# Gated linear attention with two MLP layers on one core: near score groups of the two lanes in neighbouring slots, one PSUM bank per lane

## The chip, the cores and the metric

The kernel runs on one core of a Trainium2 chip. The metric is the device time of one execution in microseconds; three executions of the kernel before gave 985.92 us (median; 984.63 to 988.6).

## The reference

```python
B, H, S, D = 4, 8, 768, 48
# attention: a state of D x D per batch and head, decayed row by row and added to
for t in range(S):
    state = alpha[:, :, t, :, None] * state + k[:, :, t] (outer) v[:, :, t]
    y[:, :, t] = q[:, :, t] @ state
# then, with the heads side by side: 3072 tokens, model 384, hidden 2048
x = y.transpose(0, 2, 1, 3).reshape(3072, 384)
h = x @ w_in;  x = (h - tanh(h)) @ w_out                                  # first MLP
h = x @ w_in;  out = (max(h, 0) + alpha * min(h, 0)) @ w_out              # second MLP
```

## The kernel before

The sequence is cut into 6 tiles of 128 steps (C); a tile with the 4 batches has 512 tokens. Tile by tile two kinds of work are interleaved: the MLP of one tile and the attention of the next. The 6 tiles of the first MLP come first (five with the attention of the next tile beside them), then the 6 of the second MLP with nothing beside them.

**The MLP.** An MLP tile is a list of 32 half slots (LAYER; here "slots"), each with 9 matmuls of 128x512 on TensorE (float32 in three products of a high and a low half). An "in" slot (0, 1, then every even one up to 28) makes one block of 128 hidden rows in the bank `ph`; an "out" slot (every odd one from 3, and 30) adds one to `acc`. After an "in" slot ACT makes the tanh, DVE the difference g (`make_g`), ACT the high half, DVE the low half (`g_low`).

**The attention.** Within a tile of 128 steps the decay is handled in 7 levels of halving (l = 1 to 7). Level by level POOL multiplies the left halves of k (`grow`, in place in `k_t`) and makes the tree of products of alpha (`product`), and DVE multiplies the right halves of q (`q_first` for the elements by alpha itself, `grow` for the levels) by totals that ACT has copied to the bank `py` (`copy_left_totals`). TensorE makes 8 groups of scores (e = 1 to 8). Groups 1 to 6 are "near": blocks of 32x32, written into one of two banks `ps`, in turns by e. DVE moves each under a mask into `near` (`mask`), and POOL places them in `prob`. Groups 7 and 8 are copied by ACT. Then come the outputs (Y, of `prob` and v and of the state), the transposes of k (KT) and the new state (ST). Group e needs k at level e - 2, q at level e - 1 and, before, mask e - 2, since that mask reads the bank that e writes.

There are 16 pairs of heads (X). A **lane** is half of them: 8 pairs (XL), 2 batches. The first tile, which has nothing to hide behind, is done lane by lane, each with two banks of scores of its own. The other five do both lanes in one group: 64 matmuls of the program for a near group, 128 in the records, since each float32 matmul is recorded twice, and as many weight loads.

**The order** beside the MLP is a table written by hand. `E_SLOT` gives the slot of each score group, and `beside()` puts masks, growth and copies of totals at or behind it. Each engine walks the same table: layer work of slot h, then the table's work of slot h. On DVE an "in" slot does `make_g` first, and an "out" slot does its `g_low` behind the table's work. What matters here:

```python
E_SLOT = {1: 4, 2: 6, 3: 9, 4: 12, 5: 15, 6: 18, 7: 21, 8: 24}
    for side in range(2):
        slots[E_SLOT[2] + 1 + side].insert(0, ("q_first", side))
```

So group 2 stands at slot 6, the two halves of `q_first` at slots 7 and 8, and group 3, which needs both, at slot 9. In the first MLP tile DVE, ACT and SP also split 12 blocks of weights (`weights`, an extra piece in each odd slot). The loads are issued by SP: `load_tile(a)` (lines 329 to 346) waits, then loads q, alpha, k and v of a tile in this order.

## Time and profile before

| what | us |
|---|---|
| three executions, median (lowest, highest) | 985.92 (984.63, 988.6) |
| the profiled execution, its own time | 993.91 |
| its span (first to last instruction) | 992.1 |
| first MLP tile with attention beside it (47.9 to 154.5) | 106.60 |
| the three in the loop | 97.40, 97.30, 95.60 |
| the fifth, without a new state | 86.70 |
| an MLP tile alone | 65.70 |

The tiles are stretches of the trace between the first matmuls of slot 0. A page of the profile gives busy time by engine (PE is TensorE's matmuls, PEld its weight loads), the granted clock in tenths, and groups of instructions by source line with their mean duration and the idle time ahead of them. "issue" is idle time for which no wait shows. A group of score matmuls in the trace has the line 432 (near), 427 (group 7) or 420 (group 8).

### The profile page before, as it was taken

How to read it: one execution, taken by the hardware profiler on the slowest of the kernel's cores; microseconds unless marked ns; L12 is line 12 of the kernel's file. 1: busy time of each engine (PE TensorE's matmuls, PEld its weight loads, DVE VectorE, ACT ScalarE, POOL GpSimd, SP SyncE). 2: the span in 40 equal slices, each digit the busy share in tenths (PEclk: the TensorE clock that was granted, in tenths of full speed). 3: DMA queues.
4: the chain of work that ended last, by engine and by line, in shares of the span. 5: the costliest groups of instructions: out<-in, count | busy, mean ns of one | idle time of the engine just before them, and what ended most of it. 6: DMA issues, size and time to landing. Idle time of an engine off the chain costs nothing.

```text
span 992.1 us, 23757 instructions
## 1 busy us (share of the span) xinstructions
PE 938.4 (95%) x10296; PEld 769.4 (78%) x10296; DVE 556.4 (56%) x695; ACT 319.2 (32%) x527; POOL 191.3 (19%) x186
## 2 busy tenths in 40 slices
PE   4688999899989998999999999999999999999998
PEld 3567778678768876887888888888888888888887
DVE  8857755564456445645653445555555555555553
ACT  4633453235323432443254452121121221211211
POOL 6422322241124112501430442000000000000000
PEclk7699999899989998999999999999999999999999
DMA  5462133004200410051004401010010010100000
GB/s 156 111 216 65 34 72 122 2 2 112 83 2 2 124 71 3 2 155 39 3 2 154 166 1 64 0 62 2 0 63 0 0 63 0 63 0 0 32 1 32
DMA packets 28999, 51.67 MB, mean 52 GB/s; under 512 B 2032, under 2 KB 19440, under 8 KB 26864
## 3 DMA queue, kind: packets, MB, share of 16 engines
q1 hardware_dynamic: 28912, 50.35, 16.7%
q8 instruction: 75, 1.23, 0.5%
q14 instruction: 12, 0.10, 0.0%
HBM read 40.90 MB, written 9.44 MB: 51 GB/s over the span
## 4 chain that ended last, share of the span: by engine, by line
PE 93%; issue 4%; DVE 2%; ACT 1%; DMA 1%; DVEq 0%; SPq 0%
PE ph L577 41%; PE acc L586 14%; PE acc L587 13%; PE acc L588 13%; PE ps L432 4%; PE py L489 1%; PE ps L420 1%; PE ps L489 1%; PE py L485 1%; PE ps L530 1%; DVE q_w L793 1%; PE ps L485 1%; DMA q_early<-q 1%; PE acc L432 1%; PE ps L427 1%
## 5 line engine op out<-in xcount | busy, mean ns | idle before, releaser
L757 ACT ACTIVATE g_hi<-g 128x512 fp32r<-128x512 f32 x192 | 121.1, 631 | 447.7 <-PE acc L588 382.9
L939 DVE TENSOR_TENSOR g_lo<-g,g_hi 128x512 fp32r<-128x512 f32 x192 | 142.1, 740 | 188.0 <-ACT g_hi L757 187.3
L586 PE MATMUL acc<-g_lo,w_hi 128*128 128x512 f32 x576 | 230.8, 401 | 0.0
L587 PE MATMUL acc<-g_hi,w_lo 128*128 128x512 f32 x576 | 225.7, 392 | 0.0
L588 PE MATMUL acc<-g_hi,w_hi 128*128 128x512 f32 x576 | 225.6, 392 | 0.0
L577 PE MATMUL ph<-x_hi,w_lo 128*128 128x512 f32 x576 | 166.9, 398 | 5.0 <-issue 2.8
L577 PE MATMUL ph<-x_hi,w_hi 128*128 128x512 f32 x576 | 164.7, 394 | 0.2 <-issue 0.2
L577 PE MATMUL ph<-x_lo,w_hi 128*128 128x512 f32 x576 | 164.5, 394 | 0.0
L925 DVE TENSOR_TENSOR g<-ph,g 128x512 f32<-128x512 f32 x96 | 66.2, 689 | 135.8 <-ACT g L738 135.5
L577 PEld LDWEIGHTS ph<-x_hi,w_lo 128*128 128x128 f32 x576 | 107.4, 190 | 29.2 <-issue 7.1
L586 PEld LDWEIGHTS acc<-g_lo,w_hi 128*128 128x128 f32 x576 | 108.9, 189 | 25.6 <-issue 2.2
L577 PEld LDWEIGHTS ph<-x_lo,w_hi 128*128 128x128 f32 x576 | 109.8, 191 | 23.7 <-issue 0.4
L577 PEld LDWEIGHTS ph<-x_hi,w_hi 128*128 128x128 f32 x576 | 109.7, 190 | 23.4
L588 PEld LDWEIGHTS acc<-g_hi,w_hi 128*128 128x128 f32 x576 | 109.1, 189 | 23.6
L587 PEld LDWEIGHTS acc<-g_hi,w_lo 128*128 128x128 f32 x576 | 109.1, 189 | 21.4
L1006 POOL TENSOR_TENSOR k_t<-k_t,tree 128x512 f32<-128x512 f32 x72 | 83.1, 1172 | 187.4 <-PE ps L432 145.9
L931 DVE TENSOR_SCALAR g<-ph,slope 128x512 f32<-128x512 f32 x96 | 72.0, 750 | 58.3 <-PE ph L577 58.3
L738 ACT ACTIVATE g<-ph 128x512 f32<-128x512 f32 x96 | 57.4, 598 | 137.7 <-PE ph L577 137.4
L432 PEld LDWEIGHTS ps<-q_w,k_t 128*32 128x32 f32 x4096 | 40.7, 112 | 37.8 <-issue 36.8
L432 PE MATMUL ps<-q_w,k_t 128*32 128x32 f32 x4096 | 45.2, 201 | 26.1 <-issue 20.6
L934 DVE SCALAR_TENSOR_TENSOR g<-ph,g 128x512 f32<-128x512 f32 x96 | 66.4, 692 | 3.3
L804 DVE TENSOR_TENSOR q_w<-q_w,py 64x1024 f32<-64x1024 f32 (+1 forms) x56 | 64.8, 1157 | 2.0 <-PE ps L432 1.1
(109 smaller groups left out, 599.6 us busy)
## 6 DMA issues: line engine op xcount, KB each, us to landing
v_t<-v SPq DMA_DIRECT2D x6, 1024.0 KB, 5.3
a_t<-alpha SPq DMA_DIRECT2D x5, 1024.0 KB, 4.9
k_t<-k SPq DMA_DIRECT2D x5, 1024.0 KB, 4.9
x<-x_out SPq DMA_DIRECT2D x6, 768.0 KB, 4.2
x_in<-x SPq DMA_DIRECT2D x6, 768.0 KB, 5.1
q_w<-q SPq DMA_DIRECT2D x10, 384.0 KB, 7.2
out<-prob SPq DMA_DIRECT2D x5, 768.0 KB, 3.8
w_raw<-w_in SPq DMA_DIRECT2D x16, 192.0 KB, 3.5
```

The lines of the kernel that those rows point to most:

```text
L432: mm = pe.matmul(at[t, NEAR * i0:NEAR * i0 + NEAR], k_t[:, x * C + t.start:x * C + t.stop], moving(x, t), start=True, stop=True)
L577: mm = pe.matmul(ph[:, f % 2, :], w[:, f, kt * 128:(kt + 1) * 128], x[:, kt, :], start=(j == 0 and kt == 0), stop=(j == 2 and kt == KT - 1))
L586: pe.matmul(acc[:, m, :], w_hi[:, f, part], g_lo[:, f % 2, :], start=(f == 0), stop=False)
L587: pe.matmul(acc[:, m, :], w_lo[:, f, part], g_hi[:, f % 2, :], start=False, stop=False)
L588: mm = pe.matmul(acc[:, m, :], w_hi[:, f, part], g_hi[:, f % 2, :], start=False, stop=(f == NF - 1))
L757: act.activation(g_hi[:, f % 2, :], g[:, f % 2, :], ACT.Copy).then_inc(g_hi_made, 1)
L804: dve.tensor_tensor(to, right, left_for_q(lane, l, rows), ALU.mult).then_inc(q_last if to_end else q_grown[set_of(lane)], 1)
L925: dve.tensor_tensor(g[:, f % 2, :], ph[:, f % 2, :], g[:, f % 2, :], ALU.subtract).then_inc(g_made, 1)
L931: dve.tensor_scalar(g[:, f % 2, :], ph[:, f % 2, :], 0.0, slope[:, f:f + 1], ALU.min, ALU.mult).then_inc(g_part, 1)
L934: dve.scalar_tensor_tensor(out=g[:, f % 2, :], in0=ph[:, f % 2, :], scalar=0.0, in1=g[:, f % 2, :], op0=ALU.max, op1=ALU.add).then_inc(g_m ...
L939: dve.tensor_tensor(g_lo[:, f % 2, :], g[:, f % 2, :], g_hi[:, f % 2, :].bitcast(F32), ALU.subtract).then_inc(g_lo_made, 1)
L1006: pool.tensor_tensor(left, left, right_totals.to_broadcast([128, XL * nb, half]), ALU.mult).then_inc(done, 1)
```

## The change

The five later tiles also work lane by lane where the scores are near. Each lane has one bank (`ps[:, lane, :]`) for all its score groups, in place of one bank for odd and one for even e. Groups 1 to 6 become two groups of half the size in neighbouring slots (lane 0 at slot h, lane 1 at h + 1); groups 7 and 8 stay in one slot, as two halves. Group 1 moves from slot 4 to 3, group 2 from 6 to 5. Masks, `q_first` and `grow` of a lane stand one slot behind its group, each of half the size; both halves of `q_first` are now in one slot. Since a lane has one bank, group e waits for mask e - 1 of its lane, and group 8 for the copies of group 7 of its lane. Copies of totals, products and placements stay together. Counters become per-lane counters. The load of q waits for the last Y of the tile before (`y_done`) rather than for `q_copied` and `q_last`.

```diff
-E_SLOT = {1: 4, 2: 6, 3: 9, 4: 12, 5: 15, 6: 18, 7: 21, 8: 24}
+E_SLOT = {1: 3, 2: 5, 3: 9, 4: 12, 5: 15, 6: 18, 7: 21, 8: 24}
...
     for e, h in E_SLOT.items():
-        slots[h].append(("scores", e))
+        for lane in range(LANES):
+            at = h + (lane if e <= 6 else 0)
+            slots[at].append(("scores", lane, e))
+            if e == 2:
+                slots[at + 1].append(("q_first", lane, 0))
+            if e > 2:
+                slots[at + 1].append(("grow", lane, e - 1))
+            if e <= 6:
+                slots[at + 1].append(("mask", lane, e))
         if e > 2:
-            slots[h].append(("left", e - 1))
-            slots[h + 1].append(("grow", e - 1))
-        if e <= 6:
-            slots[h + (1 if e == 1 else 2)].append(("mask", e))
-    for side in range(2):
-        slots[E_SLOT[2] + 1 + side].insert(0, ("q_first", side))
...
+            slots[h].append(("left", 0, e - 1))
...
-        def scores_of(lane, e):
-            if lane is None:
-                return ps[:, (e - 1) % 2, :]
-            return lane_scores[lane][(e - 1) % 2][:, 0:512 if e == 8 else 256]
+        def scores_of(a, lane, e):
+            bank = lane_scores[lane][(e - 1) % 2] if is_tile(a, 0) else ps[:, lane, :]
+            return bank[:, 0:512 if e == 8 else 256]
...
             def load_tile(a):
 
-                n = a - 1
-                if is_tile(a, 1):
-                    for lane in range(LANES):
-                        sp.wait_ge(scored[lane], SCORED)
-                else:
-                    sp.wait_ge(q_copied, 2 * n)
-                    sp.wait_ge(q_last, 2 * n)
+                sp.wait_ge(y_done, B * a)
                 for hh in range(2):
...
-                sp.wait_ge(y_done, B * a)
                 sp.dma_start(a_t[:, :], alpha[bass.ds(a * 128, 128), :]).then_inc(ld_a[LANES], 16)
...
                 if e == 2:
-                    pe.wait_ge(state_made, STATES * a)
-                    pe.wait_ge(k_grown[LANES], K_GROWN * n + K_PARTS)
-                    group(None, 2, plain(q_w, 1))
+                    pe.wait_ge(k_grown[lane], K_GROWN * a + 1)
+                    pe.wait_ge(masked[lane], MASKED * a + 1)
+                    group(a, lane, 2, plain(q_w, 1))
                     return
-                pe.wait_ge(k_grown[LANES], K_GROWN * n + K_PARTS * (e - 2))
-                pe.wait_ge(q_grown[LANES], Q_GROWN * n + 2 * (e - 1))
-                pe.wait_ge(masked[LANES], MASKED * n + e - 2)
-                if e == 8:
-                    pe.wait_ge(copied[LANES], FAR_COPIES * n + 4)
-                group(None, e, grown(e - 1))
+                pe.wait_ge(k_grown[lane], K_GROWN * a + e - 2)
+                pe.wait_ge(q_grown[lane], Q_GROWN * a + 2 * (e - 1))
+                if e < 8:
+                    pe.wait_ge(masked[lane], MASKED * a + e - 1)
+                else:
+                    pe.wait_ge(copied[lane], COPIED * a + 4)
+                group(a, lane, e, grown(e - 1))
```

How the instructions stand before and now, at three places. The rows are those of the attention beside the first MLP tile; the loop has the same order. `x32` after a row counts equal instructions of the program, and names in brackets are the counters waited for (`masked_lane0` and so on belong to a lane, names without a lane to both).

TensorE, group 3 at slots 9 and 10, before:

```order
L432 MATMUL ps<-q_w,k_t 32x32 [waits masked,q_grown,k_grown]
L432 MATMUL ps<-q_w,k_t 32x32 x63
L577 MATMUL ph<-x_hi,w_lo 128x512 [waits g_made,w_lo_made]
L577 MATMUL ph<-x_hi,w_lo 128x512 x2
L577 MATMUL ph<-x_hi,w_hi 128x512 x3
L577 MATMUL ph<-x_lo,w_hi 128x512 x3
```

and now:

```order
L426 MATMUL ps<-q_w,k_t 32x32 [waits masked_lane0,q_grown_lane0,k_grown_lane0]
L426 MATMUL ps<-q_w,k_t 32x32 x31
L573 MATMUL ph<-x_hi,w_lo 128x512 [waits g_made,w_lo_made]
L573 MATMUL ph<-x_hi,w_lo 128x512 x2
L573 MATMUL ph<-x_hi,w_hi 128x512 x3
L573 MATMUL ph<-x_lo,w_hi 128x512 x3
L426 MATMUL ps<-q_w,k_t 32x32 [waits masked_lane1,q_grown_lane1,k_grown_lane1]
L426 MATMUL ps<-q_w,k_t 32x32 x31
```

The 64 matmuls in a row became 32, nine matmuls of the MLP, and 32.

DVE, slots 6 to 8 (from group 2 to the end of `q_first`), before:

```order
L925 TENSOR_TENSOR g<-ph,g 128x512 [waits g_part]
L793 TENSOR_TENSOR q_w<-q_w,a_t 64x16x64 [waits scored,ld_a]
L793 TENSOR_TENSOR q_w<-q_w,a_t 64x16x64
L939 TENSOR_TENSOR g_lo<-g,g_hi 128x512 [waits g_hi_made]
L914 TENSOR_TENSOR w_lo<-w_raw,w_hi 128x768 [waits w_lo_made,w_hi_made]
L925 TENSOR_TENSOR g<-ph,g 128x512 [waits g_part]
L793 TENSOR_TENSOR q_w<-q_w,tree 64x16x64 [waits scored,tree_made]
L793 TENSOR_TENSOR q_w<-q_w,tree 64x16x64
L814 TENSOR_TENSOR near<-ps,near_masks 128x512 [waits masked,scored]
```

and now, slots 3 to 6 (the row of `w_lo` is in the first MLP tile alone):

```order
L922 TENSOR_TENSOR g_lo<-g,g_hi 128x512 [waits g_hi_made]
L897 TENSOR_TENSOR w_lo<-w_raw,w_hi 128x768 [waits w_lo_made,w_hi_made]
L908 TENSOR_TENSOR g<-ph,g 128x512 [waits g_part]
L798 TENSOR_TENSOR near<-ps,near_masks 128x256 [waits scored_lane0,placed_lane0,masked_lane0]
L798 TENSOR_TENSOR near<-ps,near_masks 128x256 [waits scored_lane1,placed_lane1,masked_lane1]
L922 TENSOR_TENSOR g_lo<-g,g_hi 128x512 [waits g_hi_made]
L897 TENSOR_TENSOR w_lo<-w_raw,w_hi 128x768 [waits w_lo_made,w_hi_made]
L908 TENSOR_TENSOR g<-ph,g 128x512 [waits g_part]
L779 TENSOR_TENSOR q_w<-q_w,a_t 64x8x64 [waits scored_lane0,ld_a]
L779 TENSOR_TENSOR q_w<-q_w,a_t 64x8x64
L779 TENSOR_TENSOR q_w<-q_w,tree 64x8x64 [waits tree_made]
L779 TENSOR_TENSOR q_w<-q_w,tree 64x8x64
```

The second half of `q_first` no longer stands behind the `make_g` of slot 8; the first mask of lane 0 stands behind the `w_lo` of slot 3 and the `make_g` of slot 4.

DVE, slots 18 to 20 (behind group 6), now:

```order
L908 TENSOR_TENSOR g<-ph,g 128x512 [waits g_part]
L790 TENSOR_TENSOR q_w<-q_w,py 64x8x4x16 [waits q_grown_lane0,left_copied,scored_lane0]
L790 TENSOR_TENSOR q_w<-q_w,py 64x8x4x16
L805 COPY_PREDICATED near<-near_masks,ps 128x16x16 [waits masked_lane0,scored_lane0]
L922 TENSOR_TENSOR g_lo<-g,g_hi 128x512 [waits g_hi_made]
L897 TENSOR_TENSOR w_lo<-w_raw,w_hi 128x768 [waits w_lo_made,w_hi_made]
L908 TENSOR_TENSOR g<-ph,g 128x512 [waits g_part]
L790 TENSOR_TENSOR q_w<-q_w,py 64x8x4x16 [waits q_grown_lane1,left_copied,scored_lane1]
L790 TENSOR_TENSOR q_w<-q_w,py 64x8x4x16
L805 COPY_PREDICATED near<-near_masks,ps 128x16x16 [waits masked_lane1,scored_lane1]
```

The growth for group 7 of lane 1 now stands behind the `make_g` of slot 20; both lanes' growth stood ahead of it.

## Rows read from the trace of the kernel before

**Rows 1.** Page, part 1: busy time, share, instructions.
```profile
PE 938.4 (95%) x10296; PEld 769.4 (78%) x10296; DVE 556.4 (56%) x695; ACT 319.2 (32%) x527; POOL 191.3 (19%) x186
```
**Rows 2.** Windows by MLP tile: us, busy by engine (xinstructions), PEclk, DMA share, GB/s.
```profile
251.90:349.20 97.30, 91.73 (x1456) 74.29 (x1456) 52.24 (x61) 34.06 (x60) 25.42 (x25) 0.96 0.17 48
...
531.50:597.20 65.70, 65.70 (x290) 53.98 (x289) 29.31 (x33) 32.74 (x50) 25.70 (x14) 1.00 0.36 121
```
**Rows 3.** Timeline of PE, second loop tile, slots 9, 10: start, us, work, [idle before].
```profile
277.61 1.26 PE L432 MATMUL ps<-q_w,k_t 128*32 128x32 f32 x124 [1.83 <-DVE q_w L793]
281.31 0.32 PE L432 MATMUL ps<-q_w,k_t 128*32 128x32 f32 x4 [2.44 <-issue]
281.56 1.65 PE L577 MATMUL ph<-x_hi,w_lo 128*128 128x512 f32 x3
...
288.58 0.84 PE L577 MATMUL ph<-x_hi,w_lo 128*128 128x512 f32 x3
```
**Rows 4.** Timeline of DVE at the same place.
```profile
275.02 2.46 DVE L793 TENSOR_TENSOR q_w<-q_w,tree 64x1024 f32<-64x1024 f32 x2
```
**Rows 5.** DMA queues in 278 to 281.3 us: packets, MB, share.
```profile
q8 instruction: 1, 0.02, 2.5%
```
**Rows 6.** Page, part 3: DMA queues of the whole span.
```profile
q8 instruction: 75, 1.23, 0.5%
```
**Rows 7.** Windows at the place of rows 3, columns as in rows 2.
```profile
284.00:287.50 3.50, 3.50 (x10) 2.73 (x9) 1.06 (x2) 0.60 (x1) 0.92 (x2) 0.50 0.00 0
```
**Rows 8.** Timeline of PE: the same group in the third loop tile and in the fifth tile.
```profile
378.33 0.32 PE L432 MATMUL ps<-q_w,k_t 128*32 128x32 f32 x4 [2.16 <-issue]
378.58 1.65 PE L577 MATMUL ph<-x_hi,w_lo 128*128 128x512 f32 x3
...
384.93 0.84 PE L577 MATMUL ph<-x_hi,w_lo 128*128 128x512 f32 x3
...
470.14 1.29 PE L432 MATMUL ps<-q_w,k_t 128*32 128x32 f32 x128 [1.80 <-issue]
```
**Rows 9.** Timeline of PE: idle times of the first MLP tile.
```profile
66.94 0.38 PE L432 MATMUL ps<-q_w,k_t 128*32 128x32 f32 x19 [2.24 <-issue]
...
75.18 0.54 PE L432 MATMUL ps<-q_w,k_t 128*32 128x32 f32 x38 [2.64 <-issue]
75.64 0.53 PE L586 MATMUL acc<-g_lo,w_hi 128*128 128x512 f32 x1
...
79.38 0.88 PE L577 MATMUL ph<-x_hi,w_lo 128*128 128x512 f32 x3
...
85.48 1.29 PE L432 MATMUL ps<-q_w,k_t 128*32 128x32 f32 x128 [1.79 <-issue]
...
111.88 0.39 PE L432 MATMUL ps<-q_w,k_t 128*32 128x32 f32 x23 [2.22 <-issue]
...
127.36 1.97 PE L420 MATMUL ps<-q_w,k_t 128*64 128x128 f32 x32 [1.35 <-issue]
```
**Rows 10.** Timeline of PE: an "in" slot and a group, then an "out" slot.
```profile
260.45 0.84 PE L577 MATMUL ph<-x_hi,w_lo 128*128 128x512 f32 x3
...
263.81 0.50 PE L586 MATMUL acc<-g_lo,w_hi 128*128 128x512 f32 x1
```
**Rows 11.** Lines by form, DVE, 0 to 48 us: half-size operations.
```profile
L804 DVE TENSOR_TENSOR q_w<-q_w,py 64x512 f32<-64x512 f32 x6 | 4.1, 683 | 0.1
L821 DVE COPY_PREDICATED near<-near_masks,ps 128x256 f32<-128x256 uint32 x4 | 2.1, 513 | 0.2
```
**Rows 12.** Timeline of DVE, then PE: behind slots 20 and 21, second loop tile.
```profile
312.78 0.71 DVE L821 COPY_PREDICATED near<-near_masks,ps 128x512 f32<-128x512 uint32 x1
...
313.47 1.10 PE L427 MATMUL ps<-q_w,k_t 128*32 128x64 f32 x64
```
**Rows 13.** Timeline of ACT, first MLP tile: arrival of weights.
```profile
66.84 0.85 ACT L765 ACTIVATE w_hi<-w_raw 128x768 fp32r<-128x768 f32 x1 [4.58 <-DMA w_raw<-w_out]
```
**Rows 14.** Timeline of SP's DMA issues, second loop tile.
```profile
329.06 1.40 SPq L339 DMA_DIRECT2D q_w<-q  x2
```

More of the change, by code:

```diff
@@ L447, in first_scores @@
                     pe.wait_ge(ld_q[lane], 32)
-                    group(lane, 1, plain(q_early, 0))
+                    group(0, lane, 1, plain(q_early, 0))
                     return
@@ L451, in first_scores @@
                 if l == 2:
-                    group(lane, 2, plain(q_early, 1))
+                    group(0, lane, 2, plain(q_early, 1))
                     pe.wait_ge(pads_cleared, 2)
@@ L554, in attention @@
             def attention(work, a):
-                for what, i in work:
+                for what, lane, i in work:
                     if what == "scores":
-                        scores(a, i)
+                        scores(a, lane, i)
                     if what == "Y":
@@ L685, in attention @@
                 n = a - 1
-                for what, i in work:
+                for what, lane, i in work:
                     if what == "left":
@@ L824, in mask @@
                         [128, count, nb, half]),
-                    scores_of(lane, e).rearrange("p (h n t) -> p h n t", h=count, t=half)).then_inc(done, 1)
+                    scores_of(a, lane, e).rearrange("p (h n t) -> p h n t", h=count, t=half)).then_inc(masked[lane], 1)
             def place_near_first(lane):
@@ L846, in first_tile @@
                         dve.wait_ge(scored[lane], 1)
-                        mask(lane, 1)
+                        mask(0, lane, 1)
                         continue
@@ L858, in first_tile @@
                     if l < LEVELS - 1:
-                        mask(lane, l + 1)
+                        mask(0, lane, l + 1)
                     elif lane > 0:
@@ L1027, in attention @@
                 n = a - 1
-                for what, e in work:
+                for what, lane, e in work:
                     if what != "scores" or e == 2:
```

237 lines of the change are left out of this document (113 added, 124 removed).

## The prediction

> **What bounds the kernel now.** I read the page first. TensorE is busy for 95% of the span; DVE, the next engine, for 56% [rows 1]. Windows by MLP tile then show that TensorE is not at its limit everywhere: a tile with nothing beside it takes 65.70 us and is all busy, a loop tile takes 97.30 us with 91.73 busy, so 5.6 us are idle, and its mean clock is 0.96 [rows 2]. The change adds and removes no arithmetic on TensorE, so what it can give is in the idle time and in the lost clock. The timeline of TensorE shows where they lie in a loop tile: all at group 3. TensorE waits 1.83 us for DVE's `q_first`, runs 124 of the group's 128 matmuls, stands still for another 2.44 us for which no wait shows ("issue"), and then runs two slots slowly [rows 3].
>
> The first wait has a plain cause: the second half of `q_first` takes 2.46 us on DVE and could start only at 275.02, behind the `make_g` of slot 8 [rows 4].
>
> The second stop is the arrival of code, as I read it. One packet of the instruction queue falls into it [rows 5]. Over the span the queue moved 75 packets and 1.23 MB, 16.4 KB each [rows 6], against 20,592 recorded matmuls and weight loads [rows 1], about 275 for a packet. A near group is 256 such records in 1.26 us, nearly a whole packet's worth. From the end of the wait to the last four matmuls 3.70 us pass (281.31 less 277.61) [rows 3]; if a packet needs up to that long from its cause to its use, TensorE reads such a group faster than the next packet can come. The Trainium skill ("Runtime: NRT & Kernel Launch", Instruction fetch mechanics) speaks of blocks of 16 KiB, or 256 instructions, and says that crossing into one is "mostly hidden". The size agrees with the rows above; the second half speaks against my reading, and what follows from it is a rival below.
>
> The third loss is the clock. Behind these stops it is 0.50, the 1.2 GHz level [rows 7]. The two slots behind group 3 take 7.02 us (281.56 to 288.58) [rows 3] in place of 4.1 (two of 65.70 / 32) [rows 2], so 2.9 us are lost.
>
> **What goes.** I count by tile in the profiled execution.
> - `q_first`. 1.83 us in each of the three loop tiles [rows 3], 1.79 in the first MLP tile [rows 9], 1.80 in the fifth [rows 8]: 9.1 us. Now lane 0's four pieces start behind the `make_g` of slot 6. DVE is free of a `make_g` 1.4 us behind the slot (slot 20: 312.78, and the slot ended a slot's 2.1 us before 313.47 [rows 12]); four pieces of half size cost about 0.68 each [rows 11] (the nearest form), 2.7 us, so they end 4.1 us behind slot 6. TensorE needs them after half a group (0.65) and three slots (6.2), at 6.8. Lane 1 ends at 4.1 + 0.45 (mask) + 2.7 = 7.3, needed at 6.8 + 0.65 + 2.05 = 9.5. Both are covered by more than 2 us of MLP work. Without that cover the wait would be what it was.
> - Code. 2.44 in the first and second loop tile (the first has the rows of the second) [rows 3], 2.16 in the third [rows 8], and in the first MLP tile 2.24, 2.64 and 2.22, each inside a near group [rows 9]: 14.1 us. Groups are now 128 records with a slot between: 256 records span at least two half groups and a slot, 1.3 + 2.05 = 3.3 us. Against 3.7 that leaves 0 to 0.4 us at an unlucky place. I take 0.5 us for the whole kernel.
> - Clock. 2.9 us in the second loop tile, 2.2 (6.35 less 4.1) in the third [rows 8], about as much in the first, 1.7 in the first MLP tile (75.64 to 79.38, less 2.05) [rows 9]: 9.1 us.
> - Group 8 in the first MLP tile waited 1.35 us for a late growth [rows 9]. Each lane's growth is now half as long, and lane 1 has lane 0's matmuls as cover: 1.3 us go.
>
> **What comes.**
> - Group 7, lane 1. It waits for the growth and for mask 6 of its lane, both behind the `make_g` of slot 20. In the trace DVE is free of that `make_g` at 312.78 [rows 12]. Two growths of 0.68 and a mask of 0.45 to 0.51 [rows 11] end at 314.6. Group 7 began at 313.47, and its second half could begin at 314.0 (half of 1.10 on) [rows 12]. So TensorE waits 0.6 us, in five tiles: 3.1 us. What stands behind it on DVE, `g_low`, is not needed for two slots.
> - More seams. A near group costs 3.36 us with its slot [rows 10], 1.31 more than the slot; the 128 matmuls themselves need no more than 1.26. The seam is 0.05 at least; from the form of the half groups nothing shows it. I take 0.1 and bound it by 0.25. Six more per tile, five tiles: 3.0 us (1.5 to 7.5).
> - Group 2 of lane 0 in the first MLP tile. It newly waits for mask 1, and that mask stands on DVE behind `w_lo` of slot 3, which waits for ACT, which waits for weights that arrive at 66.84 [rows 13]. Moved to slot 3, group 1 no longer hides this: TensorE reaches group 2 at about 66.9, ACT is done at 67.7, `w_lo` takes 1.0 to 2.1, `make_g` 0.7, the mask 0.45: 69.8 to 70.9. I take 3.0 us (2.9 to 4.0), and none for a slow clock behind it.
> - Masks are now in the way of each lane's next group, since a lane has one bank. At slots 4 to 20 mask and growth end 3.3 us behind an "in" slot, and the next group of that lane comes 4.1 us or more behind it, group 7 excepted. 0 us; the cover is 0.8 us at the tightest.
> - DVE: per level four half-size growths (2.7 us) in place of two (2.5), so 0.2 to 0.6 more with the masks. ACT: four more small copies for group 7. POOL has the same pieces. All lie beside MLP work: 0.
> - The load of q, issued at 329.06 [rows 14], is moved behind the last Y, some 9 us, and alpha's two issues later (1.4 us of issue). TensorE needs q and k again some 19 us behind that. 0 us; the queues have the time.
>
> **The sum.** 9.1 + 14.1 + 9.1 + 1.3 = 33.6 go; 0.5 + 3.1 + 3.0 + 3.0 = 9.6 come. On the profiled execution, 993.91 us, that is minus 24.0: 969.9. This execution is 8.0 us above the median of the three runs. No view shows what the extra is, but the lost clock is the only term that need not be there in each run: I take 7 of its 9.1, so minus 21.9 and **964.0 us** against the median of 985.92. With the outer values (clock 0 to 9.1, seams 1.5 to 7.5, group 2 2.9 to 4.0) the result is 961.9 - 1.5 = 960.4 at best, and 971.0 + 5.5 = 976.5 at worst.
>
> **Rivals.**
> - **The unexplained stops stay.** If the six "issue" stops are not code that comes late, halves of groups cure nothing, and they move to another group. Then 14.1 us are kept, and half of the clock with them, and the gain is 21.9 - 14.1 - 3.5 = 4.3, so 981.6. Against it: all six stand inside groups of 256 records, and one packet of code falls into the one that I looked at [rows 3, 5, 9]. A milder form, in which half stay, gives 973. This is the case that the Trainium skill's "mostly hidden" (the page and section above) would give.
> - **One bank per lane makes DVE the bound (slower).** Each group of a lane now waits for the mask before it. The cover is 0.8 us at groups 5 and 6. If each DVE piece behind `make_g` were late by 2 us (contention with POOL, or waits for both lanes), 10 of the 12 near half groups would wait about 1.2 us, 12 us in a tile and 60 in five: 985.9 - 21.9 + 60, over 1020. It decides from a delay of 0.8 us; at 1.2 us of delay (0.4 a group, 20 us) the gain is just eaten. For it: DVE is 56% busy and its order is rigid. Against it: in the first tile these very half-size pieces took 0.68 and 0.51 with POOL running [rows 11].
> - **The clock falls elsewhere.** The 3 us at group 2 could lower the clock, 1.7 us as in rows 9, and the timed runs may never have had the drops in the loop: 971 to 973.
>
> **Chances.** 0.62 for the forecast (959 to 971). 0.17 for half the stops, or the clock term near 0 (971 to 976). 0.12 for a small gain, 976 to 984, above all by the stops that stay, of which 0.05 within 0.5% (about 5 us, what a measurement of this kernel can tell from no change). 0.05 more for no change by DVE eating the gain. 0.04 for slower. So faster 0.86, same 0.10, slower 0.04. Range 956 to 977.
>
> **What would show it.** Right: no idle time at group 3; no "issue" gap inside a near group; PEclk 1.00 in all loop tiles; loop tiles of 90 to 92 us; about 0.6 us before the second half of group 7, with DVE named; some 3 us before group 2 in the first MLP tile, with DVE's mask named. Wrong: gaps of over 2 us inside half groups (the first rival), or many short waits for `near` (the second).

## The result: no gain, against 22 us forecast

| kernel | median, us | range, runs | ratio to the kernel before | 95% interval |
|---|---|---|---|---|
| before | 988.75 | 984.63 to 994.11, 15 | | |
| changed | 993.31 | 989.34 to 995.83, 15 | 1.0038 | 1.0021 to 1.0056 |

The changed kernel is slower by 0.4%, inside the 0.5% that I had called no change. The forecast was 964.0 us with a range of 956 to 977, so it was wrong, and wrong by mechanisms, since nearly all that I expected at group 3 did happen. The profiled execution of the changed kernel took 993.34 us (span 991.6), so both profiles stand within 1 us of one another and can be compared slot by slot.

The page of the changed kernel, part 1 (the counterpart of [rows 1]):

```profile
PE 945.5 (95%) x10296; PEld 767.3 (77%) x10296; DVE 574.0 (58%) x805; ACT 322.3 (33%) x547; POOL 198.8 (20%) x186
```

Its windows by MLP tile, the columns of [rows 2]: first tile, three loop tiles, fifth tile. (They are cut 0.18 us behind the first matmuls of slot 0, at 48.58, 152.67, 248.84, 348.08 and 442.86 us; the lengths are the same.)

```profile
48.76:152.85 104.09, 96.63 (x1537) 77.15 (x1537) 73.87 (x100) 44.55 (x77) 30.47 (x25) 0.98 0.36 97
152.85:249.02 96.17, 90.89 (x1457) 72.29 (x1457) 55.23 (x84) 36.61 (x67) 29.25 (x26) 0.99 0.22 69
249.02:348.26 99.24, 93.62 (x1457) 74.28 (x1458) 55.02 (x83) 35.02 (x64) 27.35 (x25) 0.96 0.17 49
348.26:443.04 94.78, 93.34 (x1457) 74.33 (x1458) 54.73 (x83) 33.45 (x61) 25.50 (x24) 0.97 0.14 36
443.04:531.08 88.04, 87.18 (x1377) 69.39 (x1377) 52.29 (x78) 33.01 (x60) 26.86 (x25) 1.00 0.09 33
```

The same five tiles of the kernel before, in its trace:

```profile
47.91:154.38 106.47, 95.88 (x1536) 78.09 (x1537) 70.30 (x76) 43.65 (x73) 31.87 (x26) 0.97 0.38 105
154.38:251.88 97.50, 91.25 (x1457) 73.73 (x1455) 53.00 (x64) 36.08 (x63) 25.43 (x25) 0.96 0.21 58
251.88:349.21 97.33, 91.75 (x1456) 74.31 (x1457) 52.25 (x61) 34.07 (x60) 25.42 (x25) 0.96 0.17 49
349.21:444.64 95.43, 91.13 (x1456) 73.97 (x1457) 51.01 (x61) 33.44 (x59) 25.44 (x25) 0.96 0.17 47
444.64:531.37 86.73, 84.86 (x1377) 69.18 (x1376) 48.04 (x57) 32.48 (x56) 23.69 (x24) 1.00 0.06 21
```

The loop tiles should have come to 90 to 92 us. They take 96.2, 99.2 and 94.8, where they took 97.5, 97.3 and 95.4. The second one became slower although its idle time at group 3 is gone. So something of the same size came. TensorE's waits in the tiles with attention beside them show what went and what came. The view gives, for 60 to 520 us, what was waited for, the sum in us, the number of times and the longest. Before, and then the changed kernel ("..." stands for the rows of group 8):

```profile
PE ps L432 <- issue: 17.7, 8, 2.6
PE ps L432 <- DVE q_w L793: 5.5, 3, 1.8
PE ph L577 <- issue: 3.0, 3, 1.7
...
```
```profile
PE ph L573 <- issue: 8.0, 2, 4.2
PE ps L421 <- DVE near L805: 3.3, 5, 0.7
PE ps L426 <- issue: 2.5, 2, 2.1
PE py L482 <- DVE a_t L790: 2.4, 3, 0.8
PE py L482 <- issue: 1.7, 2, 1.5
PE ps L426 <- DVE near L798: 1.4, 1, 1.4
...
PE ps L426 <- DVE near L805: 0.7, 1, 0.7
```

The 17.7 us of near groups (L432) with no releaser named are two things. Two of the eight, 1.79 and 1.80 us, stand in front of group 3 in the first and the fifth tile and are the wait for `q_first`, as the prediction counts them. The other six, 14.1 us, stand inside groups; of those 2.5 us are left (L426), and the 9.1 us of `q_first` (5.5 with DVE named, 3.6 without) are gone. New are 8.0 us in two stops of about 4 us in front of an "in" slot (`ph`), 3.3 us at group 7, 2.4 us in front of Y with DVE named and 1.7 without, and 2.1 us for masks in the first tile. The timeline of TensorE in the changed kernel shows the second of the two large stops. It stands between the last matmul of slot 31 and slot 0 of the next tile, which is where TensorE's loop jumps back:

```profile
343.51 0.39 PE L584 MATMUL acc<-g_hi,w_hi 128*128 128x512 f32 x1
348.08 1.64 PE L573 MATMUL ph<-x_hi,w_lo 128*128 128x512 f32 x3 [4.18 <-issue]
349.52 1.48 PE L573 MATMUL ph<-x_hi,w_hi 128*128 128x512 f32 x3
350.80 1.48 PE L573 MATMUL ph<-x_lo,w_hi 128*128 128x512 f32 x3
352.08 1.40 PE L573 MATMUL ph<-x_hi,w_lo 128*128 128x512 f32 x3
353.31 0.85 PE L573 MATMUL ph<-x_hi,w_hi 128*128 128x512 f32 x3
```

In the kernel before the same jump cost 1.12 us (the first one 1.68) and no clock:

```profile
347.70 0.39 PE L588 MATMUL acc<-g_hi,w_hi 128*128 128x512 f32 x1
349.21 0.96 PE L577 MATMUL ph<-x_hi,w_lo 128*128 128x512 f32 x3 [1.12 <-issue]
350.01 0.85 PE L577 MATMUL ph<-x_hi,w_hi 128*128 128x512 f32 x3
```

For the rest of the text I take lengths of slots from the same timelines, as the distance from the first matmul of one slot to that of the next. The table has the second loop tile, with slots 0 and 1 of the third for the jump.

| slots | what stands there | before | changed | difference |
|---|---|---|---|---|
| 3 to 8 | groups 1, 2 | 15.33 | 16.09 | +0.8 |
| 9 to 11 | group 3 | 15.01 | 7.97 | -7.0 |
| 12 to 20 | groups 4 to 6 | 22.76 | 23.88 | +1.1 |
| 21 to 25 | groups 7, 8 | 13.86 | 14.44 | +0.6 |
| 27 | Y | 6.92 | 7.76 | +0.8 |
| 31, 0, 1 | jump back | 7.65 | 13.12 | +5.5 |

### The profile page after: what moved, and what is told of

Its sections match the earlier page's. It is cut to its first block, busy times and chain, and to the rows that moved or that the text cites. A ratio compares the mean times of both kernels' runs of the same rounds, so it can differ in the third digit from the quotient of the medians.

```text
span 991.6 us, 24066 instructions
## 1 busy us (share of the span) xinstructions
PE 945.5 (95%) x10296; PEld 767.3 (77%) x10296; DVE 574.0 (58%) x805; ACT 322.3 (33%) x547; POOL 198.8 (20%) x186
## 4 chain that ended last, share of the span: by engine, by line
PE 86%; DVE 5%; issue 4%; ACT 3%; DMA 1%; DVEq 0%; SPq 0%; ACTq 0%
PE ph L573 39%; PE acc L582 13%; PE acc L584 12%; PE acc L583 12%; PE ps L426 4%; DVE q_w L790 2%; PE py L486 1%; DVE q_w L779 1%; PE ps L486 1%; PE py L482 1%; PE ps L526 1%; ACT prob L642 1%; DVE a_t L790 1%; DMA w_raw<-w_out 1%; PE ps L482 1%
## 5 line engine op out<-in xcount | busy, mean ns | idle before, releaser
L922 DVE TENSOR_TENSOR g_lo<-g,g_hi 128x512 fp32r<-128x512 f32 x192 | 148.7, 775 | 180.6 <-ACT g_hi L743 180.2
L573 PE MATMUL ph<-x_hi,w_lo 128*128 128x512 f32 x576 | 169.6, 403 | 10.2 <-issue 8.0
L573 PEld LDWEIGHTS ph<-x_hi,w_lo 128*128 128x128 f32 x576 | 106.2, 191 | 33.7 <-issue 12.4
L989 POOL TENSOR_TENSOR k_t<-k_t,tree 128x512 f32<-128x512 f32 x72 | 89.6, 1247 | 168.4 <-PE ps L426 137.1
L790 DVE TENSOR_TENSOR q_w<-q_w,py 64x512 f32<-64x512 f32 x106 | 72.4, 683 | 1.8
L426 PEld LDWEIGHTS ps<-q_w,k_t 128*32 128x32 f32 x4096 | 43.1, 112 | 29.9 <-issue 29.9
L426 PE MATMUL ps<-q_w,k_t 128*32 128x32 f32 x4096 | 50.4, 201 | 7.8 <-issue 5.2
## 6 DMA issues: line engine op xcount, KB each, us to landing
k_t<-k SPq DMA_DIRECT2D x5, 1024.0 KB, 10.4
```

The costliest lines, as they stand in the source:

```text
L426: mm = pe.matmul(at[t, NEAR * i0:NEAR * i0 + NEAR], k_t[:, x * C + t.start:x * C + t.stop], moving(x, t), start=True, stop=True)
L573: mm = pe.matmul(ph[:, f % 2, :], w[:, f, kt * 128:(kt + 1) * 128], x[:, kt, :], start=(j == 0 and kt == 0), stop=(j == 2 and kt == KT - 1))
L790: dve.tensor_tensor(to, right, left_for_q(a, lane, l, rows), ALU.mult).then_inc(q_grown[lane] if l < LEVELS else q_last, 1)
L922: dve.tensor_tensor(g_lo[:, f % 2, :], g[:, f % 2, :], g_hi[:, f % 2, :].bitcast(F32), ALU.subtract).then_inc(g_lo_made, 1)
L989: pool.tensor_tensor(left, left, right_totals.to_broadcast([128, XL * nb, half]), ALU.mult).then_inc(k_grown[lane], 1)
```

## The experiments

Twelve runs, in three batches that each had its own runs of the kernel before (medians 990.14, 990.43 and 990.74 us). Kernels whose name begins with b_ start from the kernel before, those with a_ from the changed one.

### 1. TensorE's loop written out, in both kernels

```diff
-            with eng.Fori(1, TILES - 2) as i:
-                tile_before_last(i, BESIDE)
+            if eng is nc.tensor:
+                for i in range(1, TILES - 2):
+                    tile_before_last(i, BESIDE)
+            else:
+                with eng.Fori(1, TILES - 2) as i:
+                    tile_before_last(i, BESIDE)
```

> The changed kernel with the same loop written out on TensorE. Theory (half of what the change should have given is lost at the jump back, which costs 3.8 and 4.2 us of idle time and then a slow clock, about 6.5 us more in slots 31, 0 and 1 at each of two seams than a tile without a jump): 10 to 13 us faster than the changed kernel, so 980 to 984. Rival (that idle time is a wait for ACT or DVE that would come anyway at the tile's seam): under 3 us faster.

> The kernel before with the loop over three MLP tiles written out on TensorE alone (the other engines keep their loops), so that there is no jump back. Theory (a jump back costs a fetch of code): the 1.1 to 1.7 us idle at the two tile seams go, 2 to 3 us in all; the stops at group 3 may move, since register instructions fall away. Rival (the idle time at the seam is register work or a wait): it stays.

Measured: the changed kernel written out takes 978.45 us, ratio 0.9870 (0.9835 to 0.9906); the kernel before written out 984.40, ratio 0.9935 (0.9903 to 0.9968). The changed kernel gains about 15 us by it, the kernel before 6, where I had expected 2 to 3; by slots 3.4 of the 6 lie at the two jumps. The profile of the changed one written out, where the jump was:

```profile
336.40 0.40 PE L588 MATMUL acc<-g_hi,w_hi 128*128 128x512 f32 x1
336.63 0.85 PE L577 MATMUL ph<-x_hi,w_lo 128*128 128x512 f32 x3
```

No stop and no slow clock. Its three loop tiles take 91.6 us each, inside my 90 to 92. So what the changed kernel gains at group 3 is real, and the jump back eats it. In the kernel before, some standstills stay with the loop written out. The same view of waits has `PE ps L436 <- issue: 16.7, 8, 2.7`, but five of the eight, 9.9 us, stand in front of group 3 and are, or contain, the wait for `q_first`; three, 6.9 us, stand inside groups. They lie at other places: the second loop tile has none and takes 90.13 us, the third has one inside group 4 and one in front of the slot behind group 3 (1.56 us) and takes 98.23.

### 2. Parts: earlier slots alone, moved code alone

The first of these is the kernel before with groups 1 and 2 at the changed kernel's slots and nothing else; the second adds 64 instructions to TensorE's program, ahead of the first MLP slot, that only wait for what is long there, so that all later code lies 64 instructions further on.

```diff
-E_SLOT = {1: 4, 2: 6, 3: 9, 4: 12, 5: 15, 6: 18, 7: 21, 8: 24}
+E_SLOT = {1: 3, 2: 5, 3: 9, 4: 12, 5: 15, 6: 18, 7: 21, 8: 24}
```

> The kernel before with one part of the change alone: groups 1 and 2 one slot earlier (slots 3 and 5), both lanes still together. Theory (the losses at group 3 hang together: the wait for q_first makes the stop for code, both make the slow clock, and the change's gain is eaten by other terms): the wait of 1.8 us goes or shrinks below 0.5, the 2.4 us stop goes with it, the granted clock stays 1.00 in the loop, slots 9 and 10 take about 5.6 us in place of 12.0, and with no new seams the timed runs are 12 to 20 us faster than before. Rival (the timed runs never had the drops and stops that the profile shows): slots 9 and 10 shrink in the profile, but the timed runs gain under 9 us, the five waits for q_first alone.

> The kernel before with 64 wait instructions that are already met (two waits each) on TensorE's queue before the first MLP slot, where TensorE idles. Nothing else moves, but all later code lies 64 instructions further on. Theory (the 2.44 us stop is code that comes late, where one packet of code lies wholly in one near group): the stop inside group 3 goes in the loop, the 1.83 us for q_first stays, the clock stays high, 4 to 5 us per loop tile less; in the first MLP tile the stops in groups 1, 2 and 6 go or move. The jump back may cost another amount than 1.1 to 1.7 us. Rival (not code): 124 + 4 matmuls with 2.2 to 2.4 us between them, as before.

Measured: earlier slots alone give 977.67 us, ratio 0.9847 (0.9787 to 0.9907, four runs, which differ by up to 13 us). The padding gives 995.88, ratio 1.0064 (1.0035 to 1.0093), of which some 5 us are the padding itself, in front of the first slot (it begins at 54.02 us, in the other kernels between 47.91 and 50.56). Group 3 in the first loop tile, timeline of TensorE, first with earlier slots, then with the padding:

```profile
181.96 1.26 PE L432 MATMUL ps<-q_w,k_t 128*32 128x32 f32 x124 [0.25 <-DVE q_w L793]
185.65 0.26 PE L432 MATMUL ps<-q_w,k_t 128*32 128x32 f32 x4 [2.44 <-issue]
```
```profile
181.07 1.29 PE L432 MATMUL ps<-q_w,k_t 128*32 128x32 f32 x128 [1.83 <-DVE q_w L799]
```

The two losses of group 3 come apart. Earlier slots take away the wait for `q_first` (1.83 to 0.25) and leave the standstill after 124 matmuls; moved code takes away the standstill and leaves the wait. A standstill that goes away when nothing but the place of the code changes is a matter of code, as I had read it. It is not cured by that: with the padding, stops came back elsewhere, 2.06 us inside group 4 of the fifth tile, 1.60 us in front of a Y batch, and 2.96 and 2.65 us at the jumps back, where the kernel before has 1.68 and 1.12. Earlier slots alone have a price too: the first tile takes 109.22 us in place of 106.47, with a stop of 3.89 us inside group 1.

### 3. What a seam costs

Group 4 of every tile cut in two halves, in slots 12 and 13, in the kernel before; same bank, same semaphore, no wait added, the DVE work of the group one slot later:

```diff
-            slots[h + 1].append(("grow", e - 1))
-        if e <= 6:
-            slots[h + (1 if e == 1 else 2)].append(("mask", e))
+            slots[h + (2 if e == 4 else 1)].append(("grow", e - 1))
+        if e == 4:
+            slots[h + 1].append(("rest", 4))
+        if e <= 6:
+            slots[h + (1 if e == 1 else 3 if e == 4 else 2)].append(("mask", e))
...
+                    if what == "rest":
+                        group(None, i, grown(i - 1), slice(XL, X))
```

> The kernel before with one group of scores, group 4 of every tile, cut in half: 64 of its matmuls in half slot 12 as before, 64 in half slot 13; same bank, same semaphore, no added wait, the number of TensorE instructions unchanged; VectorE's growth and mask after it one half slot later. Theory (the cost of a seam is TensorE's own, in going from 128x512 matmuls to the small ones and back once more): half slots 12 to 14 take 7.96 us instead of 7.59 in every tile that has the group, +0.37 a group, +1.9 us over the five tiles, with no idle time before either half, and the time is before's plus about 2 us. Rival (the 0.37 us comes from the waits on each lane's own semaphores, or from the bank of scores for each lane): half slots 12 to 14 stay at 7.59 us and the time does not move.

And the opposite, on the changed kernel with the loop written out: both halves of groups 1 and 3 back to back.

```diff
-                    if what == "scores":
+                    if what == "scores" and not (lane == 1 and i in (1, 3)):
                         scores(a, lane, i)
+                    if what == "scores" and lane == 0 and i in (1, 3):
+                        scores(a, 1, i)
```

> The changed kernel with TensorE's loop written out, and groups 1 and 3 of TensorE's list with both lanes' halves back to back (half slots 3 and 9), every other engine as it is. Theory (a seam costs TensorE 0.37 us): half slots 9 to 11 take 7.59 us instead of 7.97, half slots 3 to 7 13.67 instead of 14.04, a loop tile 90.8 instead of 91.55, and the time is that of the changed kernel with the loop written out less 3 to 4 us, about 975. Rival 1 (halves of 64 small matmuls are what lets TensorE's code arrive in time): a standstill of 2.4 us with no releaser, and half clock behind it, comes back inside group 3 or 1 in at least one of the loop tiles, +4 to 5 us each time, and the time is 977 to 985. Rival 2 (the 0.37 us belongs to the lanes' waits): nothing moves, 978.

Measured, slots: with group 4 cut, slots 12 to 14 take 2.82, 2.97 and 2.17 us in every one of the five tiles, 7.96 in place of 7.59. That is +0.37 for a seam, with no wait, no lane and no second bank involved. The run as a whole took 1008.61 us, ratio 1.0159 (1.0105 to 1.0214), where I had expected +2: with its growth one slot later group 5 waited 1.8 us or more for it in each of the five tiles, some 10 us. The stops inside groups are seven with 15.7 us, against six with 14.1; the new one, 2.21 us and a slow slot behind it, stands in the fifth tile. So the time of that run says nothing about seams, its slots do.

The joined version took 979.24 us, the same as without joining: its loop tiles are 0.3 us shorter each, its first tile 2.8 us longer. Slots 3 to 7 fell by 0.3 us, as expected. Slots 9 to 11 stayed at 7.97: the seam went, and lane 1 now has to wait for the mask of its group before, as at group 7. The two halves, timeline of TensorE:

```profile
272.88 0.76 PE L430 MATMUL ps<-q_w,k_t 128*32 128x32 f32 x64
273.83 0.75 PE L430 MATMUL ps<-q_w,k_t 128*32 128x32 f32 x64 [0.19 <-DVE near L804]
```

The second half begins 0.95 us after the first; in a group of 128 that runs through in 1.26 us it would be 0.63. A lane with one bank must have its mask done, and it pays either in a seam or in a wait. The run has a second result: groups 1 and 3, again 128 matmuls with no slot between, had no standstill in any of the three loop tiles. In the first tile the joined group 1 did have one, of 2.57 us, behind a wait of 1.47 us for DVE.

### 4. The load of q

The changed kernel also lets SP wait for all four Y batches before it loads q for the next tile. I had priced this at nothing. Done alone, in the kernel before:

```diff
-                n = a - 1
-                if is_tile(a, 1):
-                    for lane in range(LANES):
-                        sp.wait_ge(scored[lane], SCORED)
-                else:
-                    sp.wait_ge(q_copied, 2 * n)
-                    sp.wait_ge(q_last, 2 * n)
+                sp.wait_ge(y_done, B * a)
                 for hh in range(2):
                     sp.dma_start(q_w[64 * hh:64 * hh + D, :, hh, :],
...
-                sp.wait_ge(y_done, B * a)
                 sp.dma_start(a_t[:, :], alpha[bass.ds(a * 128, 128), :]).then_inc(ld_a[LANES], 16)
```

> The kernel before with one edit of the change alone: the load of q for the next tile waits for all four Y batches, as those of alpha do. Theory (the load is hidden either way): alpha and k land later behind q's packets (9 to 10 us after issue instead of 5), no TensorE wait names a DMA, all half slots of the tiles keep their lengths, and the time stays within 2 us of before. Rival (the later landing takes part in the loss at the jump back of the loop): half slots 31, 0 and 1 grow from 4.04, 2.16 and 2.04 us toward the 6.2, 4.0 and 2.75 us of the changed kernel, and the time grows by up to 9 us.

Measured: 1000.12 us, ratio 1.0092 (1.0068 to 1.0116), 9.7 us slower than before. My own theory for this run, that the load is hidden, fell; the rival held. Slots 31, 0 and 1 went to 6.28, 3.72 and 2.07 at the first jump and 6.26, 4.00 and 2.80 at the second, from 4.04, 2.16, 2.04 and 3.45, 2.16, 2.04. The three jump slots grew by 3.8 and 5.4 us, 9.2 in all, as much as the timed runs show. The other slots of the loop tiles are the same to 0.1 us but for slots 9 to 11 and 28, behind or at standstills, which moved by up to 1 us and came out 2.5 us shorter in sum. With a first tile that is 2.7 us shorter as well, the profiled execution itself is only 5.9 us above that of before (999.79 against 993.91), so the 9.7 rest on the timed runs and the place of the loss on the slots. And the reverse, the changed kernel with q loaded as before (`q_last` counts once a tile, behind lane 1's growth, so that the old wait can be written):

```diff
-                sp.wait_ge(y_done, B * a)
+                n = a - 1
+                if is_tile(a, 1):
+                    for lane in range(LANES):
+                        sp.wait_ge(scored[lane], SCORED)
+                else:
+                    sp.wait_ge(q_copied, 2 * n)
+                    sp.wait_ge(q_last, 2 * n)
                 for hh in range(2):
...
+                sp.wait_ge(y_done, B * a)
                 sp.dma_start(a_t[:, :], alpha[bass.ds(a * 128, 128), :]).then_inc(ld_a[LANES], 16)
```

> The changed kernel with the load of q for the next tile back where the kernel before has it: it waits for q's last growth and q's copy of its own tile, not for all four Y batches; q_last is counted once a tile, behind lane 1's growth. Theory (the later load of q piles the transfers of q, alpha, k and v onto the jump back of TensorE's loop, and the code that TensorE needs there comes late through full DMA engines): half slots 31, 0 and 1 at the two jumps fall from 6.2 to 6.5, 4.0 and 2.7 us to about 4.0, 2.16 and 2.04, 10 us in all, and the time is 983 to 985. Rival 1 (the jump is dear because of where its code lies, 22 instructions further than before): those half slots keep their lengths, alpha lands in 5 us again, and the time stays at 993. Rival 2 (both in part): 987 to 990.

Measured: 983.85 us, ratio 0.9937 (0.9914 to 0.9961), 9.5 us under the changed kernel's 993.31. The slots at the jump fell to 3.83, 2.17, 2.04 and 3.61, 2.19, 2.04. Both directions agree in size, on two kernels whose TensorE code differs, and each leaves TensorE's own instructions as they were, but for the value of one wait in a_load (that for `q_last`). The changed kernel and a_load were timed in different batches; by their ratios to the kernel before, 1.0038 and 0.9937, the difference is 10 us. The mechanism stands in SP's issues and in the DMA queues. Issues of the changed kernel, second loop tile, as in [rows 14], then those with q early:

```profile
334.23 1.39 SPq L336 DMA_DIRECT2D q_w<-q  x2
335.82 0.48 SPq L339 DMA_DIRECT2D a_t<-alpha  x1
338.01 0.33 SPq L341 DMA_DIRECT2D k_t<-k  x1
341.67 0.33 SPq L330 DMA_DIRECT2D v_t<-v  x1
345.67 0.42 SPq L357 DMA_DIRECT2D x<-x_out  x1
```
```profile
317.62 1.40 SPq L342 DMA_DIRECT2D q_w<-q  x2
327.86 0.35 SPq L346 DMA_DIRECT2D a_t<-alpha  x1
331.64 0.33 SPq L348 DMA_DIRECT2D k_t<-k  x1
335.30 0.33 SPq L330 DMA_DIRECT2D v_t<-v  x1
```

The 7 us around the jump, the columns of [rows 2]: changed kernel, then with q early.

```profile
343.50:350.50 7.00, 2.81 (x8) 1.94 (x7) 0.69 (x2) 1.57 (x3) 1.89 (x1) 0.71 1.00 408
```
```profile
334.00:341.00 7.00, 5.72 (x75) 4.56 (x71) 4.71 (x5) 1.58 (x3) 0.96 (x1) 1.00 0.86 309
```

With q late, q's two transfers, alpha, k, v and the store are issued within 12 us of one another. All 16 DMA engines are busy all the time (share 1.00), and alpha, k and v, which landed 4.9, 4.9 and 5.3 us after issue (page, part 6), now take 8.9, 10.4 and 9.1. No data of TensorE's is late by that: beside the MLP none of its waits names a DMA. But code comes through the same engines, and at the jump it is needed at once. With q early the engines have gaps (0.86) and TensorE stands still for less: its longest stop in front of `ph` is 1.5 us in the view of waits (`PE ph L580 <- issue: 2.8, 2, 1.5`), not 4.2.

The packets of the instruction queue show it directly. The one ahead of the second jump, DMA queues in 346.5 to 347.5 us of the kernel before, in 345.2 to 346.4 of the changed one, and in 350.5 to 351.7 of the kernel before with q late:

```profile
q8 instruction: 1, 0.02, 5.8%
```
```profile
q8 instruction: 1, 0.02, 5.6%
```
```profile
q8 instruction: 1, 0.02, 5.6%
```

The shares make 0.93, 1.08 and 1.08 us of one engine's time, so the packet itself hardly takes longer. TensorE's last matmul ends at 348.09, 343.90 and 349.45 us and slot 0 begins at 349.21, 348.08 and 353.38: before, the packet starts 1.6 us ahead of TensorE's end, and with q late 1.35 and 1.1 us behind it. In the records of the queue TensorE starts again 1.70 to 1.75 us after the end of such a packet at all 18 jumps of the nine looped kernels without padding. The queue does not name the engine that a packet is for; the fixed distance to TensorE's restart does. So what the late load does is to push the start of this packet back, by 2.0 to 2.9 us at the two jumps of the two kernels. What holds it up before it starts, no view names. The Trainium skill ("Runtime: NRT & Kernel Launch", Instruction fetch mechanics) says that a taken branch to a page outside the current window forces a fetch before execution can go on. The trace agrees: a stop at both jumps of every looped kernel and none with the loop written out. That the length of this stop depends on the loads in flight stands on these two runs. It is not the only thing that it depends on: with the padding of section 2, q early and the share at 0.82 over the 7 us around the second jump, the stops were 2.96 and 2.65 us, and the packet ahead of them took 2.1 to 2.3 us.

### 5. v behind the store

```diff
                 sp.dma_start(k_t[:, :], k[bass.ds(a * 128, 128), :]).then_inc(ld_k[LANES], 16)
-                load_v(a)
...
                 store_x(i)
+                load_v(i + 2)
```

> The kernel before with the load of v for the tile after next put behind the store of the tile that has just ended, so that v's 1 MB isn't in flight when TensorE jumps back. Theory (full DMA engines delay the code at the jump): half slots 31 and 0 at the two jumps fall from 4.04 and 3.45, and 2.16, toward the 2.17 and 2.04 us of the written-out loop, 3 to 4 us in all, and the time is 986 to 988 where before has 990; nothing waits for v. Rival (the jump back costs about 2 us by itself): no half slot changes, the time stays within 1 us.

> The changed kernel with both edits: q loaded early, v behind the store. Theory (transfers in flight at the jump): 2 to 4 us less than with q loaded early alone, 980 to 983, near the 978.5 of the written-out loop. Rival (place of the code): as the changed kernel, 993.

Measured: 988.51 us, ratio 0.9980 (0.9956 to 1.0003), and 985.46, ratio 0.9955 (0.9936 to 0.9975). Slot 31 took 3.67 and 3.41 us, and 3.46 and 3.42, in place of 4.04 and 3.45, and 3.83 and 3.61: at most 0.4 us a jump, where I expected 1.5 and more, and no gain in the time that the intervals show. A miss. Full DMA engines make the jump dear, but some 1.2 us of it (slot 31 at 3.4 against 2.17) stay when v is out of the way; whether alpha, k or the store hold these up, or the jump costs them by itself, was not tried.

### 6. Candidates that beat both kernels

Two versions with both lanes together as before, q early as before, and groups 1 and 2 at slots 3 and 5 in all tiles but the first: one with TensorE's loop written out (b_best), one with the loop kept and v behind the store (b_early_vlate).

```diff
+    at = {**E_SLOT, 1: 3, 2: 5} if early else E_SLOT
+    for e, h in at.items():
...
+        slots[at[2] + 1 + side].insert(0, ("q_first", side))
...
+BESIDE_FIRST = beside(early=False)
```

> The kernel before (both lanes together, two banks) with TensorE's loop written out, and groups 1 and 2 at half slots 3 and 5 in the tiles after the first and at 4 and 6 in the first. Theory (q_first's wait of 1.8 us goes by the earlier slots alone, the jump back by the written-out loop, and seams are what the split costs): the three loop tiles take 88.6 us each where no standstill of the code falls into a group, the fifth 85.1, the first 101.9; with one or two standstills of 2.4 to 4.5 us left, as the same kernel without earlier slots has them, the time is 974 to 980, at or under the changed kernel with its loop written out (978.5). Rival (the split and the bank for each lane are needed for the gain): the time is not under 984.

> The kernel before, its loop not written out, with groups 1 and 2 at half slots 3 and 5 in all tiles but the first, and v behind the store. A candidate for the best version. Theory: the loop tiles as with earlier slots alone (94.9, 90.2, 92.9 us) less 1 to 2 us at each jump, the first tile 106.5 or less in place of 109.2: 971 to 975. Rival (the standstills only move to other groups with the code): 977 or more.

Measured: 976.53 us, ratio 0.9883 (0.9843 to 0.9923), and 975.99, ratio 0.9858 (0.9807 to 0.9908). Both beat the kernel before by 14 to 15 us and the changed one by about 17, without a split and with two banks for both lanes; against the written-out changed kernel (978.45) they are not told apart. In b_best the second loop tile, free of standstills, takes 88.5 us, as expected. The view of waits has `PE ps L438 <- issue: 12.4, 9, 2.9`; five of the nine stand in front of group 3 (2.89 us in the first tile, 0.2 in the others), four, 8.6 us, inside groups, and one more of 2.11 us stands in front of the slot behind group 3. So the next gain would be there. For b_early_vlate I had expected 971 to 975; what v behind the store adds to earlier slots cannot be told from these four runs and the four of b_early.

## Why the prediction was wrong

Step by step, by its own terms:

- **The load of q, "0 us; the queues have the time".** This is the step that failed. It asked only when TensorE needs the data, and found 19 us of room; it did not ask what else shares the DMA engines in the stretch into which four loads were pushed. Measured by itself: +9.7 us in one kernel, -9.5 when undone in the other. It alone turns a gain of 7 us (983.85 against 990.74) into a small loss. What the runs showed in its place: the load pushes the code for the jump back, and TensorE stands 3.8 and 4.2 us there and is slow for two slots behind.
- **The base.** The forecast started from a median of three, 985.92; fifteen gave 988.75, so 2.8 us of the miss are the base. That the extra of the profiled execution was lost clock is borne out in part: of 27 timed runs of the kernel before, the nine with a granted clock of 0.973 or less have a median of 991.22 us, the ten with 0.976 or more 988.36.
- **The jump back of the loop had no term.** The rows of before showed it (1.12 us at 349.21), and I read only the stops inside groups. Written out, the changed kernel is at 978.45.
- **Seams, 0.1 us each (bound 0.25).** They cost 0.37 each, measured in slots 12 to 14 with nothing else changed, 30 of them: 11.1 us in place of 3.0. My argument was that 128 matmuls need 1.26 us and a group costs 1.31 more than its slot. It missed that the slot behind the group is longer as well: the group with the slots on both sides costs 3.36 + 2.19 less two slots of 2.04, 1.47 us in all. That was in the trace. Less the 1.26 of the matmuls it would still have given only 0.21; that a group cut in two costs 0.37 more needed the run.
- **Group 7, lane 1: 0.6 us.** Right. The row of the changed kernel, the half of lane 1:

```profile
309.17 0.65 PE L421 MATMUL ps<-q_w,k_t 128*32 128x64 f32 x32 [0.65 <-DVE near L805]
```

- **Y had no term.** Slot 27 is 1.3 us longer in the first tile, 0.8 in the loop tiles and 0.26 in the fifth. TensorE waits there for the last growth of q, which now ends 2.35 us behind the start of the slot, and before 1.56 (second loop tile). With the loop written out it is 0.3 in the loop tiles too, although DVE's last growth ends at the same distance from TensorE's last matmul ahead of Y. The half microsecond between is thus tied to the loop on TensorE. I would put it down to the values of the added waits, which a loop must compute; no run took these waits away, so that stays open. In a_load, where `q_last` is counted once a tile and waited for at another value, the slot is 7.50 us in place of 7.76, half of the way to the 7.21 of the written-out loop; but that run moves the load as well.
- **`q_first`, 9.1 us to go, and masks at nothing.** Right in the loop and the fifth tile: no wait at groups 1 to 6 there. In the first tile a mask holds up group 4 by 0.7 us. Group 8 there gave 0.4 us (slot 24: 5.45 to 5.06), not 1.3; the row that I took for a late growth names no releaser. In slots 9 to 11 of the loop tiles 6.4, 7.0 and 6.1 us went, 19.5 in all, and 1.5 in the fifth; with the seam of 0.37 a tile added back, 20.6 in the loop, this is close to the 19.9 that `q_first`, code and clock together were to give there.
- **Code, 14.1 us to go and 0.5 left.** In the loop's groups all of it went. In the first tile stops of 2.09 and 0.44 us stay inside half groups. The reading was right that the stops are code that arrives late, but my rule for the cure (128 records at a time, with a slot between) was not what decides: groups of 128 with no slot between ran through in the loop tiles of the joined version (one in its first tile did not), and 2.09 us were lost inside a half group here. With q loaded early and TensorE's instructions the same but for one wait's value, that stop is not there either (`PE ps L433 <- DVE near L806: 2.4, 1, 2.4`, and no "issue" at all at a near group). So the place of the code and the transfers in flight both move these stops; by which rule, the runs do not settle.
- **Group 2 of lane 0 in the first tile, 3.0 us.** 1.35 us, with DVE's mask named, behind a stop of 2.09 that had let DVE catch up. Where that stop is not, with q early, it is 2.4. The mechanism was right, the size a little high.
- **DVE, ACT and POOL at nothing.** Right: DVE is busier by 17.6 us over the span and nothing waits for it but what is named above. The slower rival, one bank per lane with DVE as the bound, did not come: no chain of short waits for `near` beyond group 7.

The balance closes within 2 us. On profiled executions the forecast was minus 24.0. Seams cost 8.1 more than I had, and Y 2.5 (1.3, three times 0.3, 0.26). The written-out loop saves 3.4 at the jumps that I had not counted on (8.24 + 7.65 before, less 12.52). That makes minus 16.8; the changed kernel written out has minus 15.3 (978.65 against 993.91). Its five tiles have minus 16.4, and its first MLP tile begins 1.3 us later, a start that varies from run to run. That the tiles fit so well is in part luck: the first, with its stop and its waits for masks, is 2.3 us worse than these terms say, and the other four are 1.9 better, above all in slots 24 and 28, for which I had no term. In timed runs the changed kernel written out is 11.7 us under the kernel before (978.45 against 990.14), the profiled execution of before having been one of the longer ones. From there to the changed kernel as it is, 14.7 us, the slots give 13.5 at the two jumps (26.05 against 12.52) and 1.6 at Y.

None of my rivals named what happened, though one was near it: "the clock falls elsewhere" has the slow triples behind the jump (1.64, 1.48, 1.48 us), as an effect of a stop that I had not seen coming.

## What to carry to other kernels

Price a moved load twice: by when its data is needed, and by what else runs on the DMA engines in the stretch it moves into, TensorE's own code among it, above all at a loop's jump back. Before cutting a burst of small matmuls in two, measure the burst with the slots on both sides; the price of entering and leaving it was 0.37 us here, beside 1.26 us of matmuls. And take a change apart before keeping it: here the earlier slots alone (977.67 us) gave more than the whole.

## What the runs showed of the hardware

- Code contends with data transfers. With the DMA share at 1.00 over the 7 us around a jump back, the jump stops TensorE for 3.8 and 4.2 us and leaves it at half clock for about 5 us more; with 0.86 and q early it stops for at most 1.5 us, in the kernel before for 1.1 and 1.7. The packet of the instruction queue ahead of the restart starts 2.0 to 2.9 us later against TensorE's end, takes about 1 us in both cases, and TensorE restarts 1.7 us behind its end.
- One more change from 128x512 matmuls to a burst of small ones and back costs TensorE 0.37 us, the work being the same.
- Moving TensorE's code by 64 instructions, without changing what is done, took away the six stops of 2.2 to 2.6 us inside near groups, put one of 2.1 us into another group, and made the jumps back cost 3.0 and 2.7 us in place of 1.7 and 1.1; single tiles of the same work took 90.1 to 98.2 us in one execution.
